# Block-sparse attention and two gated layers on one core: another order for the attention steps

## The reference, cut to what matters

```python
# attention: 2 batches x 8 heads, 768 positions, head size 64; block 32, window 16
k_sum = k.reshape(B, H, nb, block, D).max(axis=3)      # 24 block maxima of K
v_sum = v.reshape(B, H, nb, block, D).mean(axis=3)     # 24 block means of V
scores_l = where(|i - j| < 16, scale * q @ k.T, -1e9)  # local
scores_s = scale * q @ k_sum.T + log(block)            # summary
a = softmax(concat(scores_l, scores_s));  x = a @ concat(v, v_sum)
# layer 1 on x as (2, 768, 512)
h = relu(x @ w_in)                                     # 512 -> 1024
gate = sigmoid(conv of width 3 over positions, conv_w, of h);  x = (h * gate) @ w_out
# layer 2
xn = (x - mean) / sqrt(var + 1e-6) * g_ln
out = x + relu(xn @ w_ch1) @ w_ch2                     # 512 -> 2048 -> 512
```

## Time and profile before

| | |
|---|---|
| median of three runs | 480.55 us |
| the profiled execution | 480.42 us, of which the span of its instructions is 478.7 us |
| PE busy | 464.8 us (97% of the span) |
| DVE, ACT, POOL busy | 278.8, 210.6, 264.6 us |
| granted TensorE clock | full in every slice |
| DMA | 33.58 MB in 60677 packets, 44609 of them under 512 bytes |

### The profile page before, as it was taken

How to read it: one execution, slowest core, us unless ns; L and a number is a source line. 1 busy time by engine, 2 the same in 40 slices (tenths; PEclk the granted TensorE clock), 3 DMA queues, 4 the chain that set the end, 5 groups by cost and what they waited for, 6 DMA issues and landing times.

```text
span 478.7 us, 8262 instructions
## 1 busy us (share of the span) xinstructions
PE 464.8 (97%) x2951; PEld 416.1 (87%) x2951; DVE 278.8 (58%) x619; ACT 210.6 (44%) x516; POOL 264.6 (55%) x409
## 2 busy tenths in 40 slices
PE   7888989999999999999999999999999999999997
PEld 7777778898989988988898889899988999899985
DVE  6867677488756795985673454267563343233333
ACT  3988788834334666524533423333401331233110
POOL 3557777899801400037888777891006388878100
PEclk9999999999999999999999999999999999999999
DMA  9898952221100200000122022202020112211003
GB/s 220 176 214 211 215 136 71 60 75 47 42 0 1 88 1 0 1 0 25 65 89 88 13 77 89 66 23 89 1 110 23 43 46 88 89 48 42 0 1 131
DMA packets 60677, 33.58 MB, mean 70 GB/s; under 512 B 44609, under 2 KB 53853, under 8 KB 60637
## 3 DMA queue, kind: packets, MB, share of 16 engines
q1 hardware_dynamic: 59068, 32.66, 24.4%
q10 hardware_dynamic: 1568, 0.39, 0.4%
HBM read 28.72 MB, written 3.15 MB: 67 GB/s over the span
## 4 chain that ended last, share of the span: by engine, by line
PE 89%; SPq 6%; issue 2%; DVE 1%; POOL 1%; DMA 1%; ACT 0%; DVEq 0%; POOLq 0%
PE two L1406 9%; PE two L1407 9%; PE two L1405 9%; PE two L1382 8%; PE two L1385 8%; PE two L1384 8%; PE two L1242 5%; PE two L1244 5%; PE two L1243 5%; PE two L1312 5%; PE two L1313 5%; PE two L1311 5%; PE two L1197 2%; PE two L1227 2%; PE two L1208 2%
## 5 line engine op out<-in xcount | busy, mean ns | idle before, releaser
L1382 PE MATMUL two<-combo,wa 128*128 128x384 f32 x224 | 75.8, 338 | 0.1
L1407 PE MATMUL two<-wv,h 128*128 128x512 f32 x192 | 75.4, 393 | 0.0
L1385 PE MATMUL two<-combo,wa 128*128 128x384 f32 x224 | 75.3, 336 | 0.0
L1406 PE MATMUL two<-wv,h 128*128 128x512 f32 x192 | 75.3, 392 | 0.0
L1384 PE MATMUL two<-combo,wa 128*128 128x384 f32 x224 | 75.2, 336 | 0.0
L1405 PE MATMUL two<-wv,h 128*128 128x512 f32 x192 | 75.0, 391 | 0.0
L548 POOL TENSOR_TENSOR asum<-wst 128x256 f32<-128x256 f32 x26 | 22.8, 875 | 94.6 <-PE two L1244 50.2
L577 POOL TENSOR_TENSOR wa<-wst,wa 128x256 fp32r<-128x256 f32 x39 | 29.6, 788 | 40.8 <-ACT wa L1025 40.8
L511 POOL TENSOR_SCALAR pn<-ex,rinv 128x120 f32<-128x120 f32 x96 | 33.5, 368 | 24.3 <-DVE rinv L639 24.3
L542 POOL TENSOR_TENSOR wa<-asum,wa 128x256 fp32r<-128x256 f32 x52 | 44.2, 850 | 4.3
L1053 ACT ACTIVATE h<-u 128x384 fp32r<-128x384 f32 x32 | 16.9, 527 | 61.4 <-DVE u L851 53.7
(11 more groups left out here) (114 smaller groups left out, 1014.6 us busy)
## 6 DMA issues: line engine op xcount, KB each, us to landing
wst<-in_moe_w_ch SPq DMA_DIRECT2D x26, 512.0 KB, 3.4
vW<-in_v SPq DMA_DIRECT2D x16, 240.0 KB
kn<-in_k SPq DMA_DIRECT2D x15, 192.0 KB, 3.6
qn<-in_q SPq DMA_DIRECT2D x15, 192.0 KB, 3.7
out<-y SPq DMA_DIRECT2D x11, 256.0 KB, 2.0
wst<-in_moe_w_in SPq DMA_DIRECT2D x8, 256.0 KB, 3.1
wst<-in_moe_w_out SPq DMA_DIRECT2D x8, 256.0 KB, 2.9
vW<-vs SPq DMA_DIRECT2D x16, 72.0 KB
```

What stands on the lines that cost most here:

```text
L1382: nc.tensor.matmul(o, wk[:, 0, kk], ck[:, 0, kk], start=(first and kk == 0), stop=False, skip_group_check=True)
L1385: ins = nc.tensor.matmul(o, wk[:, 1, kk], ck[:, 0, kk], start=False, stop=(kk == 1), skip_group_check=True)
L1406: nc.tensor.matmul(o, hi, vl, start=False, stop=False, skip_group_check=True)
L1407: ins = nc.tensor.matmul(o, lo, vh, start=False, stop=(f == NFP - 1 and c == 1), skip_group_check=True)
```

## The change

The arithmetic stays. What moves:

- M(p+1) for the pairs from 2 on goes from the place after O(3p) to the place before it (for pair 7: from the step of group 18 to that of group 19). Its result is no longer put into ps_kq but into the free half of the PSUM bank in which O(3p) puts its output, so it waits for XL(3p-3), and V(p+1) waits for O(3p) to be through with the bank.
- On DVE V(p+1) goes ahead of R(3p+2) and BM(p+2), and W(p+2) follows BM(p+2) at once. The low parts of x go to the steps of the first two groups of a round, behind R(3p) in the first.
- The high part of each third group (n = 3p) is made on DVE, by a copy in front of XL(n), and no longer on ACT. The other high parts stand ahead of P in two of three steps.
- On PE Q(2) goes ahead of S(5), and on ACT and DVE the steps of groups 3 to 5 are put in another order to go with it.

The lines of the functions after the change carry other numbers, 15 more on PE, 10 more on ACT, and 1 or 3 other ones on DVE.

```diff
--- before.py
+++ after.py
@@ -199,7 +199,7 @@
         mx_done, e_done = sem("mx_done"), sem("e_done")
         ra_done, r_done, n_done = sem("ra_done"), sem("r_done"), sem("n_done")
         pt_ready, pts_done, o_ready = sem("pt_ready"), sem("pts_done"), sem("o_ready")
-        xh_done, x_done = sem("xh_done"), sem("x_done")
+        xh_done, xd_done, x_done = sem("xh_done"), sem("xd_done"), sem("x_done")
         h_ready, h_done, t0_done = sem("h_ready"), sem("h_done"), sem("t0_done")
         cv1_done, cv_done, sg_done = sem("cv1_done"), sem("cv_done"), sem("sg_done")
         gate_done, hgh_done, hg_done = sem("gate_done"), sem("hgh_done"), sem("hg_done")
@@ -250,10 +250,7 @@
         def means_at(p):
 
 
-
-            if p < 2:
-                return ps_o[p][:, GT:GT + P]
-            return ps_kq[:, 0:P] if p < NPAIR - 1 else ps_kq[:, TOK0:TOK0 + P]
+            return ps_o[1 if p == 1 else 0][:, GT:GT + P]
 
         def x_parts(n):
 
@@ -611,6 +608,7 @@
 
                 dve.wait_ge(vm_ready, p + 1)
                 if p >= 2:
+                    dve.wait_ge(o_ready, GPP * (p - 1) + 1)
                     dve.wait_ge(v_in[(p - 2) % 3], v_loads(p - 2))
                 nc.vector.tensor_copy(vs[:, p % 2], means_at(p)).then_inc(vm_done, 1)
 
@@ -640,8 +638,13 @@
 
             def x_low(n):
 
-                dve.wait_ge(xh_done, n + 1)
                 hi, lo, src = x_parts(n)
+                if n % GPP == 0:
+                    dve.wait_ge(o_ready, n + 1)
+                    nc.vector.tensor_copy(hi, src).then_inc(xd_done, 1)
+                    dve.wait_ge(xd_done, n // GPP + 1)
+                else:
+                    dve.wait_ge(xh_done, n - n // GPP)
                 nc.vector.tensor_tensor(lo, src, hi.bitcast(F32), ALU.subtract).then_inc(x_done, 1)
 
             def taps(s):
@@ -696,29 +699,34 @@
             means_out(1)
             window_keys(2)
             row_sums(3)
-            for n in range(4, NG):
+            x_low(0)
+            row_sums(4)
+            score_max(5)
+            score_max(6)
+            row_sums(5)
+            x_low(1)
+            means_out(2)
+            key_max(3)
+            window_keys(3)
+            for n in range(6, NG):
                 p, t = n // GPP, n % GPP
                 if n + 1 < NG:
                     score_max(n + 1)
-                if t == 2 and p + 2 < NPAIR:
+                if t == 0:
                     row_sums(n)
-                    key_max(p + 2)
+                    x_low(n - 4)
+                    x_low(n - 3)
+                elif t == 1:
+                    x_low(n - 3)
+                    row_sums(n)
+                elif p + 1 < NPAIR:
                     means_out(p + 1)
-                if n == 4:
-                    row_sums(4)
-                    x_low(0)
-                elif n == 5:
-                    x_low(1)
-                    x_low(2)
-                else:
-                    x_low(n - 3)
-                    if t != 2 or p + 2 >= NPAIR:
-                        row_sums(n)
-                if t == 2 and p + 2 < NPAIR:
-                    window_keys(p + 2)
+                    row_sums(n)
+                    if p + 2 < NPAIR:
+                        key_max(p + 2)
+                        window_keys(p + 2)
                 if n == COLS_STEP + 1:
                     dve.wait_ge(cols_ready, 1)
-                    means_out(NPAIR - 1)
                     nc.vector.tensor_copy(cols[:], ps_kq[:, 0:KD + 3 * KF]).then_inc(cols_done, 1)
 
                     dve.wait_ge(ktr_ready, NPAIR)
@@ -726,6 +734,8 @@
                     for c in range(2):
                         nc.vector.memset(hb[:, c, 0:1], 0.0).then_inc(pad_done, 1)
                         nc.vector.memset(hb[:, c, S + 1:S + 2], 0.0).then_inc(pad_done, 1)
+            row_sums(NG - 1)
+            x_low(NG - 4)
             x_low(NG - 3)
             dve.wait_ge(cols_done, 1)
             taps(0)
@@ -947,18 +957,23 @@
             exps(3)
             probs_out(1)
             exps(4)
-            x_high(0)
             probs_out(2)
             queries(2)
+            exps(5)
+            probs_out(3)
             x_high(1)
-            probs_out(3)
-            for n in range(5, NG):
+            x_high(2)
+            probs_out(4)
+            for n in range(6, NG):
                 p, t = n // GPP, n % GPP
                 exps(n)
-                if n == 5:
-                    x_high(2)
+                if t == 0 and n > 6:
+                    x_high(n - 2)
+                if t == 2:
+                    x_high(n - 3)
                 probs_out(n - 1)
-                x_high(n - 2)
+                if n == 7:
+                    x_high(4)
                 if t == 0 and p < NPAIR - 1:
                     queries(p + 1)
                 if n == HID_STEP + 2:
@@ -1145,6 +1160,8 @@
                 if p < 2:
                     pe.wait_ge(means_done, 1)
                     pe.wait_ge(q_done, p + 1)
+                else:
+                    pe.wait_ge(x_done, GPP * (p - 2) + 1)
                 for a in range(3):
                     for g in range(4):
                         c = MC - 2 * a - (26 if g % 2 == 0 else 0)
@@ -1161,8 +1178,6 @@
                     pe.wait_ge(ks_done, p)
                 if p >= 3:
                     pe.wait_ge(q_done, p)
-                if p >= 3:
-                    block_means(p - 1)
                 transposes(kn[:, p % 2], ps_kq, ktr_ready)
 
             def queries_t(p):
@@ -1268,12 +1283,12 @@
             for n in range(3, NG):
                 p, t = n // GPP, n % GPP
                 probs_t(n - 1)
-                if n == 3:
-                    scores(5)
                 if t == 0 and p < NPAIR - 1:
                     queries_t(p + 1)
-                if n > 3 and n + 2 < NG:
+                if n + 2 < NG:
                     scores(n + 2)
+                if t == 1 and p + 1 < NPAIR:
+                    block_means(p + 1)
                 if n >= HID_STEP:
                     pe.wait_ge(w_done, min(8 * (n - HID_STEP + 1), SPLIT_ATTN))
                     if n == HID_STEP:
@@ -1288,7 +1303,6 @@
 
                     pe.wait_ge(consts_in, 32)
                     pe.wait_ge(q_done, NPAIR)
-                    block_means(NPAIR - 1)
                     nc.tensor.transpose(ps_kq[:, 0:KD + 3 * KF], rows[:],
                                         ident[0:KD + 3 * KF, 0:KD + 3 * KF]).then_inc(cols_ready, 1)
             probs_t(NG - 1)
```

## The result

The changed kernel took 477.06 us, the median of five executions, against 480.64 us for the kernel before (five executions). One of the five, the one with the profile, was disturbed and took 1607.58 us; the other four took 476.03 to 477.94 us, with a median of 476.66. The ratio, without the disturbed one, is 0.9912 with a 95% interval of 0.9884 to 0.9940. In a second series the changed kernel took 476.91 against 480.31 us, a ratio of 0.9937 (0.9922 to 0.9953).

A forecast was written before the change was run, and what follows sets the result against it. Bound: one ring of steps across the engines, with late DMA transfers beside it. Gains of 1.92 us at O(15), 1.32 to O(18) and 0.27 at the end make 3.5 off 480.42: 476.9, median 477.0; range 475.8 to 479.3.

The forecast's parts named there:

- The ring: Round of steps from K(5) to K(6), 10.12 us: 0.79 of M and 0.53 of V and a low part leave it.
- the early order: Q(2) ahead of S(5) and new order of groups 3 to 5: hidden by the floor of O(9), so 0.
- the shared port: DVE and POOL share ports; R can lose up to 0.5 us per round to POOL's split, not counted in the sum.
- M's cover: PE idles 0.58 us ahead of O(12); M (0.79) moved there costs 0 with S earlier, otherwise 0.21.
- the slower rival: DVE's low part holds M by XL(3p-3), from a DVE lateness of 2.3 us on: 482.0 us, chance 0.10.
- The floor at O(9): Transfer of vsum(3) lands at 46.55, so O(9) cannot start before 46.73 and stays there.
- O(9) moved by more than 0.3 us: Named sign of being wrong: such a move at O(9) would show that the early order matters after all.
- The floor at O(15): Transfer of vsum(5) keeps O(15) from starting before 65.25, so it comes 1.92 us earlier than 67.17.
- The last rounds and the tail: O(15) to O(18) falls from 10.49 to 9.17 us; at T(23) one XH fewer ahead of E(23) brings 0.27.
- The high part on DVE at 0.42 us: Copy of 128x256 on DVE takes 0.42 us; cost 0 where DVE waited for PE, 0.75 per round otherwise.
- part (2): V(p+1) ahead of R and BM: 0.53 us leaves the ring; R's lateness ahead of BM costs 0.0 to 0.3.
- The first rival: The ring shrinks by half only, 0.7 us less gained per round through R and M's overhang: 478.4 us, chance 0.20.

The follow-up runs named there:

- e9_fill: Changed kernel plus ten useless transposes on PE ahead of M(3), while PE waits for v(3): 476.95 us.
- e2: Changed kernel with M(p+1) back behind O(3p): 479.37 us, ratio to the kernel before 0.9988.
- e3: Changed kernel with V(p+1) and one low part again between BM(p+2) and W(p+2): 478.26 us, ratio to the kernel before 0.9955.
- e1_again: Changed kernel run again with no edit, for a profile of an ordinary run: 476.91 us.
- e4: Changed kernel with the high part of group 3p on ACT again, with its wait for V(p+1): 477.39 us, ratio to the kernel before 0.9937.
- e6: Changed kernel with R as one instruction, the addition of 1e-9 left out: 475.63 us, ratio to the kernel before 0.9903.
- e8: Changed kernel with S(5) ahead of Q(2) on PE again: 475.95 us, ratio to the kernel before 0.9907.
- e12: Changed kernel with S(5) ahead of Q(2) and the fourth weight tile ahead of vsum(5): 479.02 us, ratio to the kernel before 0.9970.
- e10: Changed kernel without the addition of 1e-9, first weight tile ahead of vsum(0), two loads of constants behind vsum(5): 476.49 us, ratio to the kernel before 0.9911.
- e11: Changed kernel without the 1e-9 addition, first weight tile ahead of vsum(0), constants behind vsum(5), S(5) ahead of Q(2): 476.00 us.
- e7: Changed kernel with the first weight tile's two DMAs issued ahead of vsum(0): 475.72 us, ratio to the kernel before 0.9903.

## Why the prediction was right

The time, 477.0 forecast and 477.06 measured, is closer than its terms, and that is luck. The four undisturbed executions of that series have a median of 476.66, and the second series has 476.91. The ring and its two parts were right. Three other steps of the prediction were not: the floor that was to decide O(15), the early order at 0, and the shared port at 0. Their errors nearly cancel.

- **The ring.** 10.12 us with the terms 0.79 and 0.53 to lose. Right in kind and size. In e9_fill the round O(9) to O(12) was 8.79 us, the number worked out, and e2 and e3 gave 0.79 and 0.53 back in that round, one each.
- **M's cover.** Right in e9_fill, where O(12) starts 0.69 us after P(12), as before (0.68). In e1_again M ends at 56.87, O(12) starts there, and that is 0.85 us after P(12) started at 56.02: with R(12) held up, S(15) and M come late and M sticks out by some 0.17. That DVE's low part would hold M (the slower rival) is not seen: in the profile of after M waits for DVE nowhere.
- **The floor at O(9).** 46.73 forecast, 47.03 in e9_fill, behind the DMA, and 47.71 with the clock's fall, not behind it. This is the sign "O(9) moved by more than 0.3 us" that the prediction had named as one of being wrong.
- **The floor at O(15): it did not decide.** 65.25 behind a DMA was forecast; 64.97 (e9_fill) and 65.91 (e1_again) were measured, neither with a DMA wait. Without the floor the prediction's own rounds give 64.53, and e9_fill's 64.97 is that, plus 0.30 for O(9), plus 0.14 for the second round (9.15 against 9.01). So the 0.72 us that the floor put on stood in for two other delays. The floor was there, but a little below: in e9_fill vsum(5) was issued at 60.39 and not at 60.87, so that the floor worked out in the same way is 60.39 + 2.04 + 2.36 = 64.79, 0.18 ahead of O(15).
- **The last rounds and the tail.** O(15) to O(18): 9.17 forecast, 8.98 and 9.03 measured. O(18) to O(23): 14.84 before, 14.50 and 14.47 after, 0.35 for the 0.27 of the tail. The high part's move to DVE is not what brought that, since e4 takes it back and has 14.49.
- **The high part on DVE at 0.42 us.** The copy took 0.41, and e4 prices the whole part at 0.5 us or nothing.
- **R and the shared port, taken at 0: mis-sized.** R(14), which the prediction feared for, took 0.17 us after the change. R(12) meets POOL's subtraction in its new place, in e1_again:

```profile
52.30 0.73 POOL L517 TENSOR_TENSOR win<-wst,win 128x256 fp32r<-128x256 f32 x1
52.48 0.57 DVE L632 TENSOR_SCALAR ra<-rs 128x4 f32<-128x4 f32 x1
```

The one ends at 53.03, the other at 53.05. Take the profiles with M, V and the high part in their new places, and the rounds O(9) to O(12) and O(12) to O(15) less their waits for DMAs (without e6's second, where POOL waited for weights). Where the first instruction of R(12) or R(15) took 0.17 to 0.30 us, the round was 8.78 or 8.79 us (one each in e6, e8, e9 and e12, both in e10 and e11). Where it took 0.56 to 0.60 us, the round was 9.03 to 9.28 (both in e1 and e7, the second in e8, e9 and e12). In e7 BM starts 0.93 and 0.97 us after K, about the 0.92 of the prediction, and both rounds were 9.03: 0.24 us each for the hold. This is read from the rows, since no run moved POOL's split alone. In e1's first round and in e8's and e9's second BM starts 1.13 or 1.14 us after K, behind R(3p+2), which is the 0.0 to 0.3 us that part (2) counted. So e1_again's 9.16 against 8.79 is R and not the clock, which was whole by then. The first rival took this effect, with M's overhang, at 0.7 us per round; 0.24 to 0.49 happened.

- **The early order at 0.** I argued that the floor of O(9) hides it. It hides the gain, but not the loss: in e1_again a PE that came early to the queue idled 2.5 us, its clock fell, and O(9) came 0.68 us later than in e9_fill. The two spans show what the fall did in these executions: without it the span is 4.1 us shorter than before (e9_fill), with it 3.3, and 3.5 was forecast. What the part costs in the median, and how much of that is the clock, is not shown (e8, e9).

## What to carry to other kernels

Write down the ring of steps that fills a period, to the last wait, and take out what the change takes out; the sum held to 0.01 us in the round in which nothing else stood in the way, and was 0.24 us short or more in those where another engine's instruction held up a small one. Then ask where the ring will run into something fixed (a queue, a landing), and what a fast engine standing at it may lose besides the wait: on PE the clock. When a total agrees, compare the times inside it too, since here a floor that did not bind stood in for two delays that did. An edit that moves work into a shared PSUM bank carries waits for everything else that uses the bank, so its value alone and its value in the package are different numbers.

## What the runs showed of the hardware that I had not expected

Two waits of PE, 1.36 and 1.15 us with 0.86 us of work between, were followed by a granted clock of 0.50 for two microseconds and more, in full use of PE; one of 2.50 us (e4) was followed by 0.61 and 0.54 over four microseconds, and one of 1.83 us at 20 us (e10) by 0.50 again. A wait does not always bring it: e2 (1.98 us, and 1.72 at 47 us), e3 (0.77 and 1.07), e6_no_add (0.46 and 1.86), e8 (1.45), e9 (1.20), e11 (1.92 at 20 us) and e12 (0.62 and 1.57) kept a granted clock of 1.00 in their profiles. Nor is it fixed by the program, since in the same one some executions fall and others don't: e2_means_behind had seven of twelve at 0.999 or 1.000 (478.40 to 479.43 us) and four at 0.996 (480.56 to 480.70), so that a fall costs it about 1.9 us. In the changed kernel the two executions of the second series at 0.995 and 0.996 (476.79 and 477.13) lie only 0.3 to 0.6 us above the middle one at 1.000 (476.53). The kernel before falls as well: two of its 17 executions beside e9 to e12 were at 0.996, with 482.57 and 482.69 us.

Which of DVE's small instructions POOL's subtraction holds up depends on the instruction. The addition of 1e-9 on 128x4, which took 0.16 us at best, took up to 0.69; the reciprocal of the same shape took 0.17 or 0.18 us every time, also where it started inside the subtraction and had no addition ahead of it (50.64 in e6, 52.49 and 61.27 in e10, 51.68 and 60.46 in e11).
